# Retention attention into a routed MoE and a gated MLP: the first expert's weights loaded and split later, its routing cut into small portions, unused key rows not loaded

## The reference

```python
def _attn_ref(q, k, v):                       # B, H, S, D = 4, 8, 768, 64
    for t in range(S):
        state = gamma * state + einsum('bhd,bhe->bhde', k[:, :, t], v[:, :, t])
        y[:, :, t] = scale * einsum('bhd,bhde->bhe', q[:, :, t], state)

def _moe_ref(x, modality_id, w_gate, modality_bias, w1, w2):   # N, D, E, F = 3072, 512, 8, 1024
    logits = x @ w_gate + modality_bias[modality_id]
    e_idx = argmax(logits);  gate_w = softmax(logits)[e_idx]
    for e in range(E):
        h = maximum(x[e_idx == e] @ w1[e], 0)
        out[e_idx == e] = gate_w * (h @ w2[e])

def _moe2_ref(x, w_in, w_out):                # d_ff = 2048
    h = x @ w_in
    return (h / (1 + exp(-1.702 * h))) @ w_out
```

## Time and profile before

| | us |
|---|---|
| median of 3 runs | 931.2 (930.1 to 931.53) |
| the profiled execution, whole | 930.29 |
| its span in the trace | 928.5 |
| PE busy | 905.8 |
| DVE busy | 544.5 |
| ACT busy | 393.6 |
| POOL busy | 216.7 |

### The profile page before, as it was taken

One profiled execution on the slowest core, in us unless ns is written; L12 is line 12 of the kernel. 1 busy time (PEld: TensorE's weight loads), 2 busy tenths in 40 slices (PEclk: granted clock), 3 DMA queues, 4 the chain that ended last, 5 costly groups with the idle time before them and its releaser, 6 DMA issues.

```text
span 928.5 us, 18549 instructions
## 1 busy us (share of the span) xinstructions
PE 905.8 (98%) x6709; PEld 785.9 (85%) x6710; DVE 544.5 (59%) x860; ACT 393.6 (42%) x645; POOL 216.7 (23%) x231
## 2 busy tenths in 40 slices
PE   7889999999999999999999999999999999999998
PEld 5767787888888888887888899988889998889997
DVE  4697775555555552233655788644588854467663
ACT  1234423444444442233554554334555434454432
POOL 4545137632115824200120000232000021000003
PEclk9999999999999999999999999999999999999999
DMA  9999676998777876112475655687565567556553
GB/s 334 370 381 396 184 191 190 335 345 263 266 250 256 317 251 215 57 36 69 144 246 193 194 183 184 208 283 233 175 212 183 184 210 228 189 197 213 185 182 140
DMA packets 97216, 205.98 MB, mean 222 GB/s; under 512 B 7676, under 2 KB 50852, under 8 KB 97140
## 3 DMA queue, kind: packets, MB, share of 16 engines
q1 hardware_dynamic: 71056, 129.54, 42.6%
q10 hardware_dynamic: 19188, 55.64, 16.7%
q0 software_dynamic: 6896, 19.77, 6.9%
HBM read 149.04 MB, written 55.88 MB: 221 GB/s over the span
## 4 chain that ended last, share of the span: by engine, by line
PE 92%; DVE 2%; DMA 2%; issue 1%; POOL 1%; ACT 0%; ACTq 0%; POOLq 0%; SPq 0%; DVEq 0%
PE bank L1946 27%; PE bank L1948 27%; PE bank L1947 27%; PE bank L1985 2%; PE bank L1857 2%; PE bank L1828 2%; PE bank L1810 1%; PE bank L2063 1%; PE bank L1877 1%; PE bank L1866 1%; PE bank L1844 1%; DMA bias_rows<-mod_bias 1%; DMA kv_in<-kv 1%; DVE masked L1231 1%; PE bank L1891 1%
## 5 line engine op out<-in xcount | busy, mean ns | idle before, releaser
L1946 PE MATMUL bank<-ring,act_hi 128*128 128x256 f32 x672 | 190.6, 284 | 0.0
L1948 PE MATMUL bank<-ring,act_lo 128*128 128x256 f32 x672 | 190.3, 283 | 0.0
L1947 PE MATMUL bank<-ring,act_hi 128*128 128x256 f32 x672 | 190.3, 283 | 0.0
L858 ACT ACTIVATE act_hi<-act_f 128x1024 fp32r<-128x1024 f32 x84 | 88.9, 1059 | 117.6 <-PE bank L1948 117.6
L1946 PE MATMUL bank<-mix_hi,ring 128*128 128x512 f32 x336 | 131.6, 392 | 0.0
L1948 PE MATMUL bank<-mix_hi,ring 128*128 128x512 f32 x336 | 130.9, 390 | 0.0
L1947 PE MATMUL bank<-mix_lo,ring 128*128 128x512 f32 x336 | 130.8, 389 | 0.0
L1946 PEld LDWEIGHTS bank<-ring,act_hi 128*128 128x128 f32 x672 | 129.0, 192 | 0.5
L1664 DVE TENSOR_TENSOR act_lo<-act_f,act_hi 128x1024 fp32r<-128x1024 f32 x84 | 102.7, 1222 | 45.3 <-ACT act_hi L858 45.1
L1947 PEld LDWEIGHTS bank<-ring,act_hi 128*128 128x128 f32 x672 | 129.1, 192 | 0.1
L1948 PEld LDWEIGHTS bank<-ring,act_lo 128*128 128x128 f32 x672 | 129.0, 192 | 0.0
(11 more groups left out here) (246 smaller groups left out, 1508.8 us busy)
## 6 DMA issues: line engine op xcount, KB each, us to landing
ring<-w_parts SPq DMA_DIRECT2D x84, 512.0 KB, 4.5
ring<-w_parts SPq DMA_DIRECT2D x24, 1024.0 KB, 5.8
ring<-w_parts SPq DMA_DIRECT2D x24, 768.0 KB, 4.9
w_parts<-part_hi ACTq DMA_DIRECT2D x16, 896.0 KB, 4.8
qk_in<-qk SPq DMA_DIRECT2D x24, 512.0 KB, 7.7
kv_in<-kv SPq DMA_DIRECT2D x24, 512.0 KB, 8.7
raw<-w SPq DMA_DIRECT2D x24, 512.0 KB, 8.3
mix_in<-w_quads ACTq DMA_DIRECT2D x16, 512.0 KB, 4.6
```

Source lines behind the costliest of these rows:

```text
L858: copy = lambda dst, src: nc.scalar.activation(dst, src, ACT.Copy)
L1946: mm(dst, hi, w_hi, start=first, stop=False, skip_group_check=skip)
L1947: mm(dst, hi, w_lo, start=False, stop=False, skip_group_check=skip)
L1948: return mm(dst, lo, w_hi, start=False, stop=last, skip_group_check=skip)
```

## The change

The pieces 0 to 7 are issued behind the loads of tiles 17, 17, 18, 18, 21, 22, 23, 23 (they were at 13, 14, 15, 16, 19, 20, 21, 22). ACT and DVE split only pieces 0 to 4, at tiles 17 to 21. POOL splits pieces 5 to 7 behind its attention loop, once five pieces are split. The early routing goes from tiles 7 to 14 to tiles 7 to 17, in smaller portions, with `order_early` at 22 and its new second half `size_early` at 23. PE's three small products go to the ends of tiles 11, 14 and 17, and POOL's gather to tile 19. The bias is built in two portions, at tiles 2 and 3. The large one-hot of the lanes is written by two instructions. For each batch's last tile only the value rows are loaded, since nothing reads its key rows.

```diff
-EARLY_LOAD_AT = 13
-EARLY_PIECES_AT = {EARLY_LOAD_AT: (0,), 14: (1,), 15: (2,), 16: (3,), 19: (4,), 20: (5,), 21: (6,), 22: (7,)}
-EARLY_SPLIT_AT = {14: 0, 15: 1, 16: 2, 17: 3, 19: 4, 20: 5, 22: 6, 23: 7}
-EARLY_GATHER_AT = 16
+EARLY_LOAD_AT = 17
+EARLY_PIECES_AT = {EARLY_LOAD_AT: (0, 1), 18: (2, 3), 21: (4,), 22: (5,), 23: (6, 7)}
+EARLY_SPLIT_AT = {17: 0, 18: 1, 19: 2, 20: 3, 21: 4}
+ORDER_AT = 22
+COUNT_AT, CHOOSE_AT, PLACE_AT, LIST_AT = EARLY + 1, EARLY + 5, EARLY + 8, EARLY + 11
+EARLY_GATHER_AT = LIST_AT + 2
...
             def load_kv(t):
                 i = t % IN_BUFS
-                sp.dma_start(kv_in[:, i, :, :], kv[t]).then_inc(kv_landed[i], DMA_INC)
+                if t % CHUNKS < CHUNKS - 1:
+                    sp.dma_start(kv_in[:, i, :, :], kv[t]).then_inc(kv_landed[i], DMA_INC)
+                else:
+                    sp.dma_start(kv_in[:, i, 1, :], kv[t, :, 1, :]).then_inc(kv_landed[i], DMA_INC)
...
+            pool.wait_ge(w_ready, len(EARLY_SPLIT_AT))
+            for i in range(len(EARLY_SPLIT_AT), EXPERT_PIECES):
+                hi, lo = (W[:, slot_at(0) + at_:slot_at(0) + at_ + PIECE] for at_ in piece_places(i))
+                pool.wait_ge(raw_in[i % RAW_BUFS], DMA_INC * (i // RAW_BUFS + 1))
+                nc.gpsimd.tensor_copy(hi, raw[:, i % RAW_BUFS, :]).then_inc(hi_copied, 1)
+                pool.wait_ge(hi_copied, i - len(EARLY_SPLIT_AT) + 1)
+                nc.gpsimd.tensor_tensor(lo, raw[:, i % RAW_BUFS, :], hi.bitcast(F32), ALU.subtract).then_inc(w_ready, 1)
...
-                tt(e_lane_hot[:, :, :], e_lane_i[:, :].unsqueeze(2).to_broadcast([P, EARLY, P]),
-                   c_("lane").unsqueeze(1).to_broadcast([P, EARLY, P]), ALU.is_equal).then_inc(early_hot_ready, 1)
+                for i in range(0, EARLY, EARLY // 2):
+                    tiles = slice(i, i + EARLY // 2)
+                    tt(e_lane_hot[:, tiles, :], e_lane_i[:, tiles].unsqueeze(2).to_broadcast([P, EARLY // 2, P]),
+                       c_("lane").unsqueeze(1).to_broadcast([P, EARLY // 2, P]), ALU.is_equal).then_inc(early_hot_ready, 1)
...
                 if t == SETTLE_AT + 1:
                     prepare_bias()
+                    bias_of(0)
+                if t == SETTLE_AT + 2:
+                    bias_of(1)
+                if t == COUNT_AT:
+                    rate_early()
+                if t == COUNT_AT + 1:
+                    count_early()
+                if t == CHOOSE_AT:
+                    choose_early()
+                if t == CHOOSE_AT + 1:
+                    name_early()
+                if t == CHOOSE_AT + 2:
+                    rank_early()
+                if t == PLACE_AT:
+                    place_early()
+                if t == PLACE_AT + 1:
+                    tiles_early()
+                if t == PLACE_AT + 2:
+                    lanes_early()
+                if t == LIST_AT:
+                    list_early()
+                    take_early()
+                if t == ORDER_AT:
+                    order_early()
+                if t == ORDER_AT + 1:
+                    size_early()
                 if t in EARLY_SPLIT_AT:
                     first_lo(EARLY_SPLIT_AT[t])
```

More of the change, by code:

```diff
@@ L156 @@
 swapped = lambda pair: pair % 2 == 1
-EARLY_LOAD_AT = 13
-EARLY_PIECES_AT = {EARLY_LOAD_AT: (0,), 14: (1,), 15: (2,), 16: (3,), 19: (4,), 20: (5,), 21: (6,), 22: (7,)}
-EARLY_SPLIT_AT = {14: 0, 15: 1, 16: 2, 17: 3, 19: 4, 20: 5, 22: 6, 23: 7}
-assert len(EARLY_SPLIT_AT) == EXPERT_PIECES
-EARLY_GATHER_AT = 16
+EARLY_LOAD_AT = 17
[4 more added lines that the diff above has]
+EARLY_GATHER_AT = LIST_AT + 2
 EARLY_MARK = 8
@@ L720, in split_pieces @@
                     nc.gpsimd.tensor_copy(hi, raw[:, i % RAW_BUFS, :]).then_inc(hi_copied, 1)
-                    pool.wait_ge(hi_copied, EXPERT_PIECES * rank + i + 1)
+                    pool.wait_ge(hi_copied, EXPERT_PIECES * rank + (EXPERT_PIECES - len(EARLY_SPLIT_AT)) + i + 1)
                     nc.gpsimd.tensor_tensor(lo, raw[:, i % RAW_BUFS, :], hi.bitcast(F32), ALU.subtract).then_inc(w_ready, 1)
@@ L1268, in hidden_lo, with rate_early @@
                     tt(hT_lo[:, part, :], ps_hT[s], hT_hi[:, part, :].bitcast(F32), ALU.subtract).then_inc(hT_split, 1)
-            def count_early():
+            def rate_early():
                 dve.wait_ge(logits_added, EARLY // TRIPLE)
+                dve.wait_ge(tables_in, DMA_INC)
                 step(red(e_top[:, :], logits[:, 0:EARLY, :], AX_X, ALU.max))
@@ L1276, in count_early @@
                                                     c_("expert").unsqueeze(1).to_broadcast([P, EARLY, NE]), ALU.mult, ALU.add))
+            def count_early():
                 step(red(e_arg[:, :], e_val[:, :, :], AX_X, ALU.min))
@@ L1289, in choose_early, with name_early @@
                 step(tt(e_is[:, :], e_key[:, :], e_one[:, 2:3].to_broadcast([P, NE]), ALU.is_equal))
+            def name_early():
                 step(red(e_one[:, 0:1], e_count[:, :], AX_X, ALU.max))
@@ L1312, in order_early, with size_early @@
                 step(tt(e_up_to[:, :, :], e_up_to[:, :, :], e_earlier[:, :, :], ALU.add))
+            def size_early():
                 step(ts(e_earlier_slots[:, :, :], e_earlier[:, :, :], float(P), None, ALU.mult))
@@ L1326, in place_early, with tiles_early @@
                                                     ALU.mult, ALU.add))
+            def tiles_early():
                 step(nc.vector.tensor_copy(e_at_i[:, :], e_at[:, :]))
@@ L1338, in lanes_early, with take_early @@
                     early_hot_ready, 1)
-                tt(e_lane_hot[:, :, :], e_lane_i[:, :].unsqueeze(2).to_broadcast([P, EARLY, P]),
-                   c_("lane").unsqueeze(1).to_broadcast([P, EARLY, P]), ALU.is_equal).then_inc(early_hot_ready, 1)
+                for i in range(0, EARLY, EARLY // 2):
+                    tiles = slice(i, i + EARLY // 2)
+                    tt(e_lane_hot[:, tiles, :], e_lane_i[:, tiles].unsqueeze(2).to_broadcast([P, EARLY // 2, P]),
+                       c_("lane").unsqueeze(1).to_broadcast([P, EARLY // 2, P]), ALU.is_equal).then_inc(early_hot_ready, 1)
+            def take_early():
                 step(tt(e_take[:, :, :], e_is[:, :].unsqueeze(2).to_broadcast([P, NE, EARLY]),
@@ L1355, in prepare_bias, with bias_of @@
                 step(nc.vector.tensor_copy(mod_f[:, :], mod_i[:, :, 0]))
[L1356 to L1361, removed]
+            def bias_of(m):
+                step(ts(r_top[:, :], mod_f[:, :], float(m), None, ALU.is_equal))
+                dst = bias if m == 0 else r_diff
+                step(tt(dst[:, :, :], over_e(r_top[:, :]), over_t(bias_rows[:, m, :]), ALU.mult))
+                if m == NMOD - 1:
+                    step(tt(bias[:, :, :], bias[:, :, :], r_diff[:, :, :], ALU.add))
             for t in range(TILES):
@@ L1883, in parts @@
                 wait(pe, logits_summed, n)
-                if n == EARLY // TRIPLE:
+                if n == CHOOSE_AT // TRIPLE:
                     pe.wait_ge(early_count_read, 1)
-                if n == EARLY // TRIPLE + 1:
+                if n == PLACE_AT // TRIPLE:
                     pe.wait_ge(early_pos_read, 1)
-                if n == EARLY // TRIPLE + 2:
+                if n == LIST_AT // TRIPLE:
                     pe.wait_ge(early_token_ready, 1)
@@ L1923, in _ @@
                     scores(1)
-                if t == EARLY + 2:
+                if t == CHOOSE_AT:
                     pe.wait_ge(early_counted, 1)
+                    pe.wait_ge(logits_summed, t // TRIPLE)
                     mm(ps_e_count, c_("ones"), e_count[:, :], start=True, stop=True).then_inc(early_count_done, 1)
-                if t == EARLY + 5:
+                if t == PLACE_AT:
                     pe.wait_ge(early_chosen, 1)
+                    pe.wait_ge(logits_summed, t // TRIPLE)
                     mm(ps_e_pos, c_("before"), e_own[:, :], start=True, stop=False)
                     mm(ps_e_pos, c_("ones"), e_before[:, :], start=False, stop=True).then_inc(early_pos_done, 1)
-                if t == EARLY + 8:
-                    pe.wait_ge(early_hot_ready, 2)
+                if t == LIST_AT:
+                    pe.wait_ge(early_hot_ready, 3)
+                    pe.wait_ge(logits_summed, t // TRIPLE)
                     for i in range(EARLY):
```

## The result

The changed kernel takes 935.99 us (median of 9 runs, 934.23 to 941.53), the kernel before 931.53 beside it (9 runs, 927.43 to 933.32). The ratio is 1.0056, interval 1.0039 to 1.0073: slower. The forecast was 932.1, no change that can be told. The profiled execution took 935.72, its span is 933.9, so there are 5.4 us of span to find (the medians differ by 4.5).

The account below looks back on a forecast made before the run. PE's queue was taken to set everything, so only PE's pauses pay. Terms -3.0 - 0.5 + 4.4 = +0.9 us on 930.29 gave 931.2, forecast as 932.1 for the median; range 927.8 to 934.3.

Parts of the forecast that it names:

- DVE's waits and "issue" pauses, tiles 9 to 18: Attention: smaller portions remove PE's waits for DVE, 3.0 us; both DMA edits together shorten "issue" pauses by 0.5 us.
- routing beside POOL's splits: Before `turn_parts(7)`: eight DVE steps stopped by POOL's three pieces, so PE stands 4.4 us before the first expert product.
- The waits of 1.68 and 0.74 at 63 and 68 us: PE's waits for late DVE around tiles 11 and 12; splitting the routing removes both.
- The 0.57 us at 26.75: PE's early wait for DVE; `mask(4)` and `copy_parts(0)` no longer stand behind the second bias product, gaining 0.57 us.
- the lower bound that the text gave: Gain from smaller routing and bias portions: 3.0 us expected, bounds 2 and 3.5.
- two kinds of wait: PE's attention waits: those ending with DVE, 2.2 us each for `copy_parts` and `mask`, and "issue", 2.4 and 2.2 us.
- Rival A: POOL's copies do not stop DVE: loss at the end only 0.8 us, sum -2.7, 928.5 us; chance 0.18.
- SP's queue and the landings: Tile 23's loads go out near 90.5, landing by 99.2, hidden with nearly 4 us of cover: no cost.
- The gather: At tile 19 POOL's gather waits for the list while `scale` runs some tiles ahead: nothing.
- rival C: POOL starts its pieces late, behind DVE splits stopped by `scale` up to 2.3 us: 934.1 us, slower; chance 0.16.
- a wait for `scores`: Sign: this, or PE waiting in the middle of tiles 17 to 21, would show the pieces' burst was taken too lightly.

Follow-up runs that it names:

- Experiment 8: Kernel before with only the routing and the bias cut into portions; pieces, gather and POOL as before: 930.38 us, ratio 0.9978.
- experiment 4: Changed kernel plus four extra products, results unread, on a free bank just before `turn_parts(7)`: 935.67 us, a single run.
- experiment 2: Changed kernel with only POOL's gather moved two tiles later, to tile 21: 937.33 us (4 runs), ratio 1.0064.
- experiments 1: Changed kernel with `order_early` and `size_early` moved from tiles 22 and 23 to tiles 13 and 14: 931.87 us, ratio 1.0014.
- 5: Changed kernel with the last three pieces split by ACT and DVE, none by POOL; order stays at tile 22: 932.92 us, ratio 1.0011.

## Why the prediction was wrong

| term | forecast | profile |
|---|---|---|
| DVE's waits and "issue" pauses, tiles 9 to 18 | -3.0 - 0.5 | -4.25 |
| routing beside POOL's splits | +4.4 | +4.24 |
| split behind the gather, tile 20 | 0 | +4.25 |
| clock behind the last wait (its stretch) | 0 | +1.2 |
| start and rest | 0 | +1.2 - 1.2 |
| sum | +0.9 | +5.4 |

*Gain in tiles 9 to 18: right in its mechanism, and helped by luck.* The waits of 1.68 and 0.74 at 63 and 68 us shrank to 0.49 and nothing, 1.9 us. Another 1.7 us are "issue" pauses, for which the forecast had 0.5 and which differ by more than that from one kernel to the next. The 0.57 us at 26.75 went as foretold, but the first stretch got no shorter: PE waited 1.42 and 2.10 us for POOL's scalings there, with the clock at half behind the second, where it had waited 3.18. The forecast's two kinds of wait leave these out. Experiment 8 puts the portions at 2 us, the lower bound that the text gave, since part comes back as "issue".

*The loss at the end: right, in size and mechanism.* The steps go through one for each POOL instruction, and POOL's last subtract ends at 114.38 (forecast 113.8). None slips through in the short pause between a copy and its subtract, as the forecast had it for two of them; the three steps left over take only 0.6 us once POOL is done. Rival A, in which POOL's copy does not stop DVE, falls: the steps at 107.66 and 111.09 end with copies. The two sides of the Trainium skill's rule ("SBUF — State Buffer", "Who interferes with whom") that the forecast weighed, any reading GpSimd instruction and a loser that fully blocks, both agree with these rows.

*SP's queue and the landings: right for PE, not for POOL.* PE waited nowhere for a tile's data in tiles 20 to 23, although tile 23's loads went out at 93.45 and not near 90.5, since the piece ahead of them waited for the held split. But POOL waited for data, 5.04 us for tile 19.

*The gather: the step that failed.* "POOL's gather waits at tile 19 for the list, as it did at 16, and its `scale` runs some tiles ahead: nothing." POOL was not tiles ahead. It did tile 19's scaling at 81.80, late from its wait for data. The gather took it to 87.36, and four scalings had piled up behind it. They ran back to back just when DVE had a split of a piece, which the change puts into every tile from 17 to 21. PE's wait of 3.42 us for `mask` and the slow products behind it made the stretch 4.25 us longer, where the forecast had nothing. The warning stood in the trace of the kernel before. The subtract of 3.07 us was held through two POOL instructions in a row, 76.42 and 77.65, and these two stood behind the gather:

```profile
74.10 1.03 POOL L667 DMA_INDIRECT gathered<-x_rows,token_of_early  x1 [3.60 <-DVE token_of_early L1347]
```

I read the 3.07 us as "up to 2.3 us" of delay and used it only for rival C. In four profiles with the gather at tile 19 the wait of `mask` at tile 20 was 3.4, 3.1, 2.9 and 2.3 us; in the four with it at tile 21 there was none of over 0.7. Rival C, which had the sign right, put the same cause in another place. The forecast had named a wait for `scores` as the sign that the pieces' burst was taken too lightly. The burst makes POOL's data late, but it can't be the cause alone: with the gather at tile 21 POOL waited 3.7 to 5.0 us for tile 19's data too, and no long split followed. Whether the backlog would form without the burst no run tells.

*A pause priced at its own length: the second omission.* The forecast let PE stand for 4.4 us and then go on at full speed. The rows show 1.2 GHz for some 3 us after both pauses, and experiment 4 that the 1.5 us of `up(0)` are this alone. The Trainium skill ("TensorE: Matmul & The Clock Gate", "Part 1: The HAM clock gate") states that the throttled state is the default and that activity releases it. The trace agrees, 5.58 against 7.07 us for the same products. What a pause brings is not fixed, though: the clock did not fall behind 3.18 us in the kernel before and behind 2.3 us in experiment 4.

Undoing the two errors one at a time does not give their sum back. The order is worth 0.42% (4.2 + 1.5 us of the profile's terms, 3.9 us by the ratio). The gather, alone, nothing that can be seen (experiment 2). With the order right it is worth 0.2% (1.0014 to 0.9994), 1.9 us of a wait of 3.1, or 1.4 by the medians. So the wait at tile 20 is shown in its mechanism by the traces, and its price by the runs is less than the 4.25 us of the table.

**Open.** Why a split is held through two or four POOL instructions in a row at 76.71 and 87.09, and gets in at the first boundary at 94.80, no run tells. With the gather at tile 21 no split in these tiles took over 2.3 us; on the kernel before, with the gather at 16, the split behind it took 3.07 and 3.58 us in two profiles and 1.7 in two others. What the "issue" pauses are is open too. Between 50 and 117 us they come to 0.9 us in the changed kernel, to 2.4 in the one before and to 1.5 to 4.9 in the experiments; they tend to be longer where PE waits less for DVE, without strict order.

## What to carry to other kernels

Before moving small dependent steps, count the other engine's instructions that share the port, not their time: each can hold one step, so eight short steps beside six long instructions end only with the sixth. A queue that is held up at one place, by late data or a slow instruction, pays when it is released, by a burst that stops whoever needs the port; look for the victim there. Give a pause of PE like these, of 3 to 4 us, a chance of costing another 1.3 to 1.5 us by the clock. Count against the removal of a wait what the next kind of pause takes back: here about half of the gather's, and all that could be seen of it while the last wait still stood.

## What was unexpected of the hardware

- A DVE subtract of 1.2 us took 5.87 (5.88 and 5.87 again in experiments 1 and 4, 4.65 in 5), held over four POOL instructions of 4.5 us in all.
- Products whose result is dropped (four calls, eight instructions of 128x512, 3.60 us), placed inside a wait, kept the granted clock at 2.4 GHz and gave `up(0)` its 1.5 us back, though the one run of that kernel was no faster.
- Pauses of 2.10, 3.42 and 4.25 us in the changed kernel were followed by half the clock; one of 3.18 us in the kernel before and one of 2.3 us in experiment 4 were not.
- "Issue" pauses mostly grew as waits were taken away (0.9 us with 8.1 of waits for DVE, 4.3 with 4.7, 3.4 with 0.7), and were not ordered by the bytes loaded.
- The clock's fall behind 24 narrow products at 131 us in the kernel before is absent in the changed one, with the same products.
